# Moving seven idle matmuls, four small products and three copies in the opening of a fused attention and two-layer MLP kernel

## What is computed

```
for t in range(S):                       # per batch and head
    cur = outer(u * k[t], v[t])
    y[t] = r[t] @ (state + cur)
    state = w[:, None] * state + outer(k[t], v[t])
x = y as (3072, 384)
h = x @ w_in ;  g = h * tanh(softplus(h)) ;  x = g @ w_out      # layer 1
h = x @ w_in2;  g = where(h > 0, h, exp(h) - 1);  out = g @ w_out2  # layer 2
```

## Time and profile before

| | |
|---|---|
| median of three runs | 863.78 us |
| the profiled execution's own time | 863.78 us |
| its span, first to last instruction | 862.2 us |
| PE busy | 854.8 us, 99% of the span |
| DVE, ACT, POOL busy | 503.0, 380.1, 168.8 us |
| granted TensorE clock | 1.000 mean |
| chain that ended last | PE 97%, DMA 1%, DVE 1% |

### The profile page before, as it was taken

How to read it: one execution, slowest core, us unless ns; L and a number is a source line. 1 busy time by engine, 2 the same in 40 slices (tenths; PEclk the granted TensorE clock), 3 DMA queues, 4 the chain that set the end, 5 groups by cost and what they waited for, 6 DMA issues and landing times.

```text
span 862.2 us, 14255 instructions
## 1 busy us (share of the span) xinstructions
PE 854.8 (99%) x6249; PEld 708.0 (82%) x6249; DVE 503.0 (58%) x563; ACT 380.1 (44%) x402; POOL 168.8 (20%) x113
## 2 busy tenths in 40 slices
PE   9999999999999999999999999999999999999998
PEld 7887888888888888888888888888888888888886
DVE  8897766655666665554369554454554554454443
ACT  6786766566656556666697221121121121220211
POOL 3662334332324332200236200000000000000000
PEclk9999999999999999999999999999999999999999
DMA  8544331222133122202223110110110000100101
GB/s 319 193 140 144 107 140 59 63 89 63 54 96 113 58 63 89 63 2 83 91 74 128 56 36 1 38 37 0 37 37 1 36 1 1 37 0 1 37 1 36
DMA packets 20065, 56.62 MB, mean 66 GB/s; under 512 B 2976, under 2 KB 5280, under 8 KB 20000
## 3 DMA queue, kind: packets, MB, share of 16 engines
q1 hardware_dynamic: 14832, 44.87, 15.6%
q10 hardware_dynamic: 5168, 10.82, 3.6%
HBM read 44.28 MB, written 9.44 MB: 62 GB/s over the span
## 4 chain that ended last, share of the span: by engine, by line
PE 97%; DMA 1%; DVE 1%; issue 0%; POOL 0%; ACT 0%; POOLq 0%; SPq 0%
PE y_ps L870 45%; PE h_ps L813 34%; PE a_ps L813 11%; PE a_ps L670 2%; PE a_ps L647 1%; PE a_ps L660 1%; PE y_ps L677 1%; DMA mid<-in_first_T 1%; PE y_ps L813 1%; DVE win_lo L1226 0%; PE h_ps L690 0%; DMA mid<-in_w 0%; PE y_ps L718 0%; PE y_ps L723 0%; POOL mid L502 0%
## 5 line engine op out<-in xcount | busy, mean ns | idle before, releaser
L813 PE MATMUL h_ps<-x_split,win_hi 128*128 128x512 f32 (+1 forms) x864 | 265.7, 389 | 0.1
L870 PE MATMUL y_ps<-g_hi,wout_hi 128*128 128x512 f32 x576 | 224.1, 389 | 0.0
L870 PE MATMUL y_ps<-g_lo,wout_hi 128*128 128x512 f32 x576 | 224.1, 389 | 0.0
L870 PE MATMUL y_ps<-g_hi,wout_lo 128*128 128x512 f32 x576 | 224.0, 389 | 0.0
L813 PEld LDWEIGHTS h_ps<-x_split,win_hi 128*128 128x128 f32 x864 | 159.8, 188 | 33.2 <-DVE x_split L1178 0.2
L813 PE MATMUL h_ps<-x_split,win_lo 128*128 128x512 f32 (+1 forms) x432 | 166.8, 386 | 0.0
L1235 DVE TENSOR_TENSOR g_lo<-mid,g_hi 128x1024 fp32r<-128x1024 f32 x96 | 152.3, 1586 | 3.3
L1242 DVE TENSOR_TENSOR mid<-mid 128x1024 f32<-128x1024 f32 x48 | 61.6, 1284 | 141.6 <-ACT mid L993 141.6
L870 PEld LDWEIGHTS y_ps<-g_lo,wout_hi 128*128 128x128 f32 x576 | 108.1, 188 | 22.5
L870 PEld LDWEIGHTS y_ps<-g_hi,wout_lo 128*128 128x128 f32 x576 | 108.1, 188 | 22.4
L870 PEld LDWEIGHTS y_ps<-g_hi,wout_hi 128*128 128x128 f32 x576 | 108.1, 188 | 22.4
(11 more groups left out here) (135 smaller groups left out, 806.2 us busy)
## 6 DMA issues: line engine op xcount, KB each, us to landing
att<-in_att SPq DMA_DIRECT2D x20, 584.0 KB, 5.4
att<-in_att SPq DMA_DIRECT2D x20, 512.0 KB, 3.7
w_raw<-in_w_in SPq DMA_DIRECT2D x16, 384.0 KB, 3.3
w_raw<-in_w_out SPq DMA_DIRECT2D x16, 384.0 KB, 3.0
x_dram<-mid ACTq DMA_DIRECT2D x6, 768.0 KB, 3.3
att<-x_dram SPq DMA_DIRECT2D x6, 768.0 KB, 4.4
out<-mid ACTq DMA_DIRECT2D x5, 768.0 KB, 3.8
mid<-in_first_T SPq DMA_DIRECT2D x2, 512.0 KB, 5.4
```

The source lines that it names most:

```text
L813: m = nc.tensor.matmul(ps, a, b_, start=n == 0, stop=n == len(terms) - 1)
L870: m = nc.tensor.matmul(y_ps[:, o, :], a, b_, start=unit == 0 and t == 0 and j == 0, stop=unit == UNITS - 1 and t == 1 and j == 2, skip_gro ...
```

## The change

On PE, keep_warm goes from 6 and 7 to 9, 3 and 2: nine before the count, three before first_own(0), two behind it. first_own(2) moves from behind first_main(0) to behind first_main(1); first_own(3) moves from behind the scores of item 2 to between first_states(0) and first_states(1). On ACT, weight_hi(0) goes ahead of first_x_hi(0), and first_x_hi(1) ahead of the copy for first_own(2). On DVE, first_x_lo(1) goes ahead of the waits for the tables and of first_state_of(0).

```diff
             pe.wait_ge(idle_zeros, 1)
-            keep_warm(6)
+            keep_warm(9)
             pe.wait_ge(consts, 4)
             pe.wait_ge(inside_done, 1)
             nc.tensor.matmul(extra_bank[0:1, 0:1], inside_min, ones, start=True, stop=True).then_inc(count_ps, 1)
-            keep_warm(7)
+            keep_warm(3)
             first_own(0)
+            keep_warm(2)
 
             pe.wait_ge(table_done, 1)
...
             first_main(0)
-            first_own(2)
 
             pe.wait_ge(k_wide_done, 1)
...
             m.then_inc(k_pow_ps, 1)
             first_main(1)
+            first_own(2)
             first_states(0)
+            first_own(3)
             first_states(1)
             first_item_scores(2)
-            first_own(3)
             first_item_scores(3)
...
             m.then_inc(k_wide_done, 1)
+            weight_hi(0)
             first_x_hi(0)
+            first_x_hi(1)
             first_own(2)
-            weight_hi(0)
-            first_x_hi(1)
             first_fill(2, 0)
...
             first_x_lo(0)
             decay_first_k(1)
+            first_x_lo(1)
             dve.wait_ge(table_done, 1)
             dve.wait_ge(state_zeroed, 2)
             first_state_of(0)
-            first_x_lo(1)
             decay_first(3)
```

## The result

The changed kernel took 867.90 us in the median of five runs (866.32 to 870.11); before took 863.78 on the same chip. The ratio (of the means, as all ratios here) is 1.0052, 95% interval 1.0034 to 1.0070: slower by 0.5%, 4.1 us, and outside the range forecast. The five times lie 3.8 us apart, where those of before lie 1.8 apart. The profiled execution took 866.53 us, span 865.0, so it is one of the quicker ones; it is 2.8 us behind before's span.

What follows compares the result with a forecast made beforehand. PE was taken to bound the kernel. Opening terms 1.26 - 0.18 - 0.14 = 0.94 us vanish in PE's wait before item 4's scores; item 4's later load adds 0.4 to 863.78: 864.2 us, range 862.9 to 865.3.

Steps and rivals of the forecast that it cites:

- PE's clock falls back: Rival, in the opening: the gap before first_own(0) drops PE's clock, 1.4 us lost, time 865.3 to 865.8; chance 7%.
- the gap before first_own(0): PE, in the opening: about 1.1 us with nothing to do before first_own(0), which starts at 7.26 instead of 6.46.
- The count: PE's 1x1 product behind the first idle matmuls: three more move it 0.80 later, to 5.27; 1.28 if the rise is late.
- four signs of being wrong: Low-level steps after 5 us; count at 5.7 or later; item 4's scores before 30.5 or after 31.6; new PE wait 31-70 us.
- The two behind first_own(0): PE, in the opening: two idle matmuls behind first_own(0) cost 0.46 us in full, bounds 0 and 0.46.
- The moved products: first_own(2) and first_own(3) on PE: same work, sum zero; waits of 0.18 and 0.14 us go.
- the wait at 67 us: PE wait of 1.37 us at about 67 us, far behind the change, which the profile puts to no engine.
- DMA and POOL: Item 4's load lands 0.4 us later (bounds 0 and 1.05); POOL's row, DVE's release and item 4's scores follow.
- The cushion: PE's 0.89 us wait before item 4's scores, for DVE's state, absorbs about that much delay; rival it doesn't hold: 864.7, 12%.
- Other rivals: Among them: DVE, held up by POOL, misses PE, 865.7, chance 6%; DVE comes before POOL's item 5 operation, 863.7, chance 5%.
- the rival "faster": PE's unexplained wait of 1.37 us at 67 us closes: 862.8, or 862.3 if the landing costs nothing; chance 7%.

Runs made afterwards that it cites:

- e1: The kernel before with only the idle matmuls moved (9, 3 and 2 in place of 6 and 7): 867.28 us.
- e7: The kernel before with idle matmuls 9, then 7 ahead of first_own(0), then 2 behind it, old order of small products: 862.90 us.
- e2: The changed kernel with idle matmuls put back to 6 and 7, only the moves left: six executions 860.9 to 863.6 us, six 864.5 to 867.0.
- e8: The kernel before with nine idle matmuls ahead of the count, four behind it, none after first_own(0): 865.20 us.
- e9: The changed kernel with seven idle matmuls instead of three ahead of first_own(0): nine of twelve executions 865.1 to 865.6 us, three 862.1 to 862.6.
- e12: The changed kernel with seven idle matmuls ahead of first_own(0) and first_own(3) back behind the scores of item 2: 862.58 us.
- e4: The changed kernel with two more idle matmuls behind first_own(2) and two behind first_own(3): 867.37 us.
- e6: The kernel before with six idle matmuls ahead of the count, then five, and two behind first_own(0), old order: 863.30 us.
- e5: The kernel before with weight_lo(1) on DVE ahead of first_x_lo(2) instead of behind first_x_lo(3): 862.98 us.
- e10: The changed kernel with seven idle matmuls ahead of first_own(0), two more behind first_own(2) and two behind first_own(3): 865.38 us.
- e11: The kernel before with two idle matmuls added behind first_own(0) and weight_lo(1) moved on DVE into its idle time: 862.60 us, ratio 0.9990.

## Why the prediction was wrong, step by step

- **The step that failed is the rival "PE's clock falls back".** It had 7% and a price of 1.4 us. It was the result. Three things were off in it. It was said to fall behind the gap before first_own(0) or not at all; there are two places, item 0's scores behind it (e1 against e7: 9.0 us of low time against 0.0; e2 and e8 fell there without a gap) and the crowded small products (e9 against e12: 5.2 against 0.3), of which the prediction had the second in no case: "the same work elsewhere, sum zero". It was priced once and for 3 us; the changed kernel spends 9.8 us in the mean at the low level, and in e4 a fall before the small products lasted from 8 to 18 us. At 0.5 us each that is 4.9 us, or 4.2 to 4.5 over the 0.9 to 1.4 us that before spends there itself, and the measured difference is 4.1. And "no row of before shows a fall" was read from one execution: of before's 29 executions beside e1 to e4, 10 list 0.998 or 0.997. One profile can't say that falls are rare. The range was also drawn up to 865.3 as "most of the clock's case above", while that case was priced at 865.3 to 865.8, outside it.
- **The count.** Forecast 5.27, with 5.76 (1.28 later) as the bound if the rise is late. The changed kernel's profile has 5.76; of the kernels with nine ahead, six profiles have 5.75 or 5.76 and two 5.25 and 5.34 (e4, e12), so the bound was the usual case. Three of the four signs of being wrong came in the changed profile: low-level steps after 5 us, the count at 5.7 or later, and item 4's scores after 31.6 (33.88). The gap before first_own(0) was 0.66 (forecast 1.1), as the idle matmuls themselves took longer. The rule that I cited for it (the Trainium skill, "TensorE: Matmul & The Clock Gate", "Part 1: The HAM clock gate": the end of the warm-up moves from run to run) the profiles bear out: seven idle matmuls behind the count took 1.88 us before and 3.04 in e2. I should have let it change a chance, not one term.
- **The two behind first_own(0)** cost 9.21 - 8.65 = 0.56 (forecast 0.46), on the path, and bring no falls (e6); if they do anything to the clock, it is to keep it (see e8).
- **The moved products** won 0.24 in the profiled pair (forecast 0.32). Executions at 1.000 take 862.3 in e2 and e9, but the wait at 67 us has a share in that.
- **DMA and POOL.** POOL's first operation on item 4 starts at 22.09, 0.38 later (forecast 0.4), for a load issued 1.35 later. The number is right by luck. It was forecast as the load's landing, but POOL has no wait before 22.09: it comes straight from its fill for item 3 (line 492), which was forecast to end at 21.4 and ended at 22.1. The load, issued at 18.22, landed 3.6 us later at 21.8.

```profile
20.41 1.71 POOL L492 TENSOR_SCALAR_AFFINE_SELECT first_scores<-mid 128x512 f32<-128x512 f32 x2 [3.40 <-ACT mid L948]
22.09 2.37 POOL L298 TENSOR_TENSOR att<-att,pow_kr 128x1024 f32<-128x1024 f32 x1
```

- **The cushion** held where the clock did: in e7 PE waits 0.31 for the state instead of 0.89, DVE's block of weights again takes 2.44, and the time is 862.9. In the changed kernel it was used up.
- **Other rivals.** No new wait came between 31 and 70 us. The wait at 67 us didn't close in the changed kernel (0.94), but it isn't fixed: seven of the profiles don't have it, and it is 1.71 in e5. It goes with the loads of instructions, which the profile lists as a DMA queue of its own ("instruction", 16 KB a load). In all seven profiles with the wait no such load starts between 55 and 64.5 us and the next one starts at 65.3 to 68.6, 0.7 to 2.2 us ahead of the wait (before: load at 65.9, PE idle from 66.9 to 68.3). In all seven without it a load falls between 55 and 64.5. What puts that load late is open, and so is whether it is what PE waited for. (The changed kernel has one more matmul ahead of it, 14 idle ones for 13, and not two as the prediction says.)

Leaving the clock out, the forecast of 864.2 would have been too high all the same: e7 has the changed kernel's late count and two idle matmuls and stands at 862.9, e9 has the moved products besides and takes 862.3 where it lists 1.000, before 862.7 to 863.5. Neither profile has the wait at 67 us; that is the rival "faster", priced at 862.3 to 862.8 and given 7%.

What stays open: why the two small products bring a fall together and not alone (e10 didn't settle it), what part the two idle matmuls behind first_own(0) have, and what sets the wait at 67 us.

## What to carry to other kernels

An idle matmul is worth what it covers: place them so that PE has columns to stream until the very moment at which the real work is ready, also in the execution in which the rise comes late or early, for four of them too few ahead of small products cost 4 us here (e1 against e7). When small products are moved, look at what stands in a row afterwards: two harmless moves made a fall together. And list the granted clock of several executions before pricing a clock fall at a few per cent: spread between executions is the sign of it.

## What the runs showed of the hardware that was not expected

- The clock fell back with PE never still for over 0.9 us (e4), and in e9 with no recorded wait of PE at all between 1.62 and the fall at 20 us. On this point the Trainium skill, "TensorE: Matmul & The Clock Gate", section "Why this matters for your kernels", asks in a row of its table to avoid idle gaps between bursts of matmuls. That is not enough here: ahead of e9's fall PE ran matmuls of 2 and 48 columns with its busy column full.
- The fall need not be near what was edited: in e1 the too few idle matmuls end at 7.5 us, and the scores start to slow at 11.
- How long seven 128x512 matmuls take after six of the same ranged from 1.88 to 3.23 us (e11) between executions of kernels that are alike up to there.
- What DVE loses beside POOL goes by POOL's end: weight_lo(1), 0.95 us on the first block, took 2.39 to 3.04 where it started during POOL's operation on item 5, and ended 0.80 to 0.82 us after that operation in six profiles (before, e1, e6, e7, e8, e12).
